# A fused convolution, low-rank mix and spectrum kernel: the second batch's convolution placed inside the first batch's blocks

## The reference

```python
# layer 1: causal convolution of 7 taps, the taps of each of 8 heads (24 channels) softmax-normalised
w = exp(weight - max); w = w / (sum(w) + 1e-9)
out[b, s, h] = sum_k w[h, k] * x_pad[b, s + k, h]
# layer 2: a low-rank mix over the positions (rank 32), then a two-layer network
u = x + (x^T @ U @ V)^T ;  x2 = u + relu(u @ w_ch1) @ w_ch2          # 192 -> 768 -> 192
# layer 3: real part of a 2-D Fourier transform over positions and channels, then again
mixed = real(fft(fft(x2, axis=1), axis=2)) ; u = x2 + mixed
un = (u - mean) / sqrt(var + 1e-6) ;  out = u + relu(un @ w_ch1') @ w_ch2'
```

## Time and profile before

| what | value |
| --- | --- |
| median of 3 runs | 1360.45 us (1359.39 to 1361.96) |
| the profiled execution | 1360.61 us, its span 1358.8 us |
| TensorE busy | 1301.7 us (96%) |
| VectorE busy | 940.5 us (69%) |
| ScalarE busy | 714.5 us (53%) |
| GpSimd busy | 470.7 us (35%) |

### The profile page before, as it was taken

The page is one execution under the profiler, slowest core; times in us unless marked ns, Lnnn a source line. Parts: engine busy times, 40 slices in busy tenths (PEclk is TensorE's granted clock), DMA queues, the critical chain, the costliest instruction groups (busy, mean ns, idle before and its releaser), DMA issues.

```text
span 1358.8 us, 25244 instructions
## 1 busy us (share of the span) xinstructions
PE 1301.7 (96%) x9128; PEld 1262.6 (93%) x9128; DVE 940.5 (69%) x2381; ACT 714.5 (53%) x1745; POOL 470.7 (35%) x611
## 2 busy tenths in 40 slices
PE   7799997859999999999999999999999999999998
PEld 7699996749999999999999999999999999999998
DVE  7857875755786886865788786875565666665554
ACT  5246653424565665654555665654444555555553
POOL 0001633550132474651133275561011234433332
PEclk9899997979999999999999999999999999999999
DMA  9842322113224323213224323311222222322220
GB/s 273 300 128 66 108 69 91 60 52 97 65 69 149 103 80 125 80 38 105 70 66 137 104 76 130 97 41 51 66 69 78 92 73 92 101 70 80 79 80 35
DMA packets 57757, 127.21 MB, mean 94 GB/s; under 512 B 8308, under 2 KB 24316, under 8 KB 55702
## 3 DMA queue, kind: packets, MB, share of 16 engines
q1 hardware_dynamic: 53602, 119.20, 27.9%
q0 software_dynamic: 4032, 6.41, 1.5%
HBM read 84.37 MB, written 46.77 MB: 97 GB/s over the span
## 4 chain that ended last, share of the span: by engine, by line
PE 80%; DVE 10%; ACT 3%; issue 3%; DMA 3%; POOL 2%; SPq 0%; POOLq 0%; ACTq 0%; DVEq 0%
PE bank L581 17%; PE bank L582 8%; PE bank L562 7%; PE bank L570 6%; PE bank L569 6%; PE bank L566 6%; PE bank L563 6%; PE bank L615 4%; PE bank L585 3%; DVE X L1069 3%; PE bank L638 3%; PE bank L630 2%; PE bank L629 2%; DMA vraw<-in_moe_V 2%; PE bank L628 1%
## 5 line engine op out<-in xcount | busy, mean ns | idle before, releaser
L776 ACT ACTIVATE ht<-bank 128x384 fp32r<-128x384 f32 x528 | 259.0, 490 | 467.1 <-PE bank L570 466.4
L982 DVE SCALAR_TENSOR_TENSOR ht<-bank,ht 128x384 fp32r<-128x384 f32 x528 | 293.3, 555 | 287.8 <-ACT ht L776 285.4
L581 PE MATMUL bank<-w,ht 128*128 128x384 f32 x1320 | 416.2, 364 | 5.5 <-DVE ub L990 3.5
L582 PE MATMUL bank<-w,ht 128*128 128x192 f32 x1320 | 331.0, 251 | 0.0
L1218 POOL TENSOR_TENSOR ub<-ub,tmp 128x576 f32<-128x576 f32 x88 | 125.7, 1429 | 589.9 <-DVE ub L990 438.9
L581 PEld LDWEIGHTS bank<-w,ht 128*128 128x128 f32 x1320 | 248.4, 188 | 12.7 <-issue 7.3
L582 PEld LDWEIGHTS bank<-w,ht 128*128 128x128 f32 x1320 | 252.0, 191 | 0.0
L562 PE MATMUL bank<-uth,w1h 128*128 128x384 f32 x528 | 189.2, 358 | 0.5 <-ACT uth L766 0.4
L570 PE MATMUL bank<-uts,w1t 128*128 128x384 f32 x528 | 180.4, 342 | 0.0
L569 PE MATMUL bank<-uts,w1s 128*128 128x384 f32 x528 | 179.9, 341 | 0.1
L566 PE MATMUL bank<-utl,w1h 128*128 128x384 f32 x528 | 179.5, 340 | 0.0
(11 more groups left out here) (115 smaller groups left out, 2562.5 us busy)
## 6 DMA issues: line engine op xcount, KB each, us to landing
f1t<-f_copy SPq DMA_DIRECT2D x44, 396.0 KB, 3.2
x_two<-ub SPq DMA_DIRECT2D x44, 288.0 KB
ub<-x_two SPq DMA_DIRECT2D x44, 288.0 KB, 3.1
mix<-mixed SPq DMA_DIRECT2D x44, 288.0 KB, 3.3
out<-ub SPq DMA_DIRECT2D x44, 288.0 KB
xin<-in_x SPq DMA_DIRECT2D x6, 1632.0 KB
vch<-v_split SPq DMA_DIRECT2D x44, 192.0 KB, 2.6
mixed<-rowk SPq DMA_DIRECT2D x88, 74.2 KB
```

Source lines behind the costliest of these rows:

```text
L581: e.matmul(dn[t][:, 0:2 * D], hh, w2[ph][:, m, :], start=(m == 0), stop=False)
L582: mm = e.matmul(dn[t][:, 0:D], hl, w2[ph][:, m, 0:D], start=False, stop=False)
L776: e.activation(hth[q % 4], up[q % 3][:, 0:TOK], ACT.Relu).then_inc(act_h, 1)
L982: e.scalar_tensor_tensor(htl[q % 4], up[q % 3][:, 0:TOK], 0.0, hth[q % 4].bitcast(F32), ALU.max, ALU.subtract).then_inc(dve_l, 1)
```

## The change

The second batch's convolution (c = 1) moves forward: piece 0 to steps (2,1) to (4,5), piece 1 to (6,1) to (8,5), piece 2 to (9,3) to (10,4) and groups 0 to 5 of the lone spectrum stage. Loads and T parts move with it. In the spectrum stage stand now also the split of T (group 10), the low-rank and make_u of block 11 (group 14) and its turn (group 16), which before came after the stage. The last block's output is added up by VectorE there instead of GpSimd. There are three row buffers instead of two. GpSimd's adds of a piece begin as soon as the first product that they need is in the plan (`late`), for all batches. At the start V's first split stands behind the third piece's taps on VectorE, V's second split is made by GpSimd after T's split, V's raw tile lies on the memory of `xin`, `prod` and `f1t` instead of the tiles of the blocks, SyncE stores the second half and loads `f1t` later, and VectorE makes five heads of the fourth piece instead of four.

```diff
-VEC_HEADS_0 = (5, 5, 4, 4)
+VEC_HEADS_0 = (5, 5, 4, 5)
...
-ROWS = 2
+ROWS = 3
...
+        T_LAST, LOW_AT, TURN_AT = 10, 14, 16
...
             if c == 1:
-                spots = [[(n, m) for n in range(n0 + 3, n0 + 7) for m in range(M6)],
-                         [(n, m) for n in range(n0 + 8, n0 + 11) for m in range(M6)],
-                         [("s", g) for g in range(3, NG)]]
-                loads = [(n0, 0), (n0 + 7, 0), ("s", 0)]
-                parts = [(n0 + 7, 3), ("s", 1), ("s", NG)]
+                span = lambda a, z: [(v // M6, v % M6) for v in range(a[0] * M6 + a[1], z[0] * M6 + z[1])]
+                spots = [span((2, 1), (5, 0)), span((6, 1), (9, 0)),
+                         span((9, 3), (10, 5)) + [("s", g) for g in range(6)]]
+                loads = [(0, 0), (5, 0), (9, 0)]
+                parts = [(5, 3), (9, 3), ("s", 8)]
...
# SyncE, start
+            store_v(0)
+            load_v(0)
+            load_v(1)
             e.wait_ge(pe_cv, len(PIECES_0))
-            e.wait_ge(ld_f1, 16)
-            load_f1(0)
-            load_f1(1)
             load_w2(1, w2b)
...
+            store_v(1)
+            e.wait_ge(ld_f1, 16)
+            load_f1(0)
+            load_f1(1)
...
# TensorE, spectrum_alone
-                for g in range(NG + 1):
+                for g in range(NG):
                     if ("s", g) in t_part:
                         part_of_t(*t_part[("s", g)])
+                    if g == LOW_AT:
+                        low_rank(NB)
+                    if g == TURN_AT:
+                        turn(NB)
                     if g + 2 < NG:
                         group_in(0, g + 2)
-                    if g < NG:
-                        group_out(0, g)
-                for q in range(4):
-                    e.wait_ge(tb_free[q], fills[("low", NB, 0)][1] if q == 0 else fills[("low", NB, 1)][1] if q == 1
-                              else filled[q])
+                    group_out(0, g)
+                for q in (2, 3):
+                    e.wait_ge(tb_free[q], filled[q])
...
# ScalarE: t_high(1) at group 10, turned_high(NB) at group 16
# VectorE, spectrum_alone
                 add_residual(NB - 1)
+                e.wait_ge(dve_y, NB * TB)
+                e.tensor_tensor(u_slot(NB - 1), u_slot(NB - 1), tmp[:], ALU.add).then_inc(pool_y, 1)
...
+                    if g == T_LAST:
+                        t_low(1)
+                    if g == LOW_AT:
+                        make_u(NB)
+                    if g == TURN_AT:
+                        turned_low(NB)
...
# VectorE, start
             start_taps(1)
-            v_low(0)
             start_taps(2)
-            v_low(1)
+            v_low()
             start_taps(3)
...
# GpSimd
-                late = -(-(VEC_HEADS + POOL_HEADS) * steps // (VEC_HEADS + PROD_OPS)) + 1
+                first = VEC_HEADS + POOL_HEADS
+                late = min(v for v in range(steps) if first in share(VEC_HEADS + PROD_OPS, v, steps, 0, 1))
...
+            e.wait_ge(v_h, 2)
+            e.wait_ge(dve_tst, 2)
+            vh = vout[2 * R:4 * R, :].rearrange("r (j p) -> r j p", p=128)
+            e.tensor_tensor(vh, vraw[2 * R:4 * R, :].rearrange("r (p j) -> r j p", j=N2)[:, 17:N2, :],
+                            vh.bitcast(F32), ALU.subtract).then_inc(v_l2, 1)
+            e.wait_ge(v_l2, 1)
```

More of the change, by code:

```diff
@@ L119, in program @@
         X = sb("X", [128, N2, D], F32)
+        with nc.sbuf_tensor("vraw", [4 * R, S], F32) as vraw:
+            pass
         xin = sb("xin", [128, PW + PAD, D], F32)
@@ L143, in program @@
         ident = sb("ident", [128, 128], F32)
-        with nc.sbuf_tensor("vraw", [4 * R, S], F32) as vraw:
-            pass
         uth = sb("uth", [128, 2, TOK], F32R)
@@ L290, in program @@
         for n in range(LAST + 1):
-            if n == 0 or previous(n) is None:
+            if n == 0:
                 fill_low(n)
@@ L309, in program @@
                     fill(("in", 0, g), (0, 2)[g % 2], True)
-                for g in range(NG + 1):
+                for g in range(NG):
                     if ("s", g) in t_part:
                         fill(("t",) + t_part[("s", g)], 0, False)
+                    if g == LOW_AT:
+                        fill_low(NB)
+                    if g == TURN_AT:
+                        fill_turn(NB)
                     if g + 2 < NG:
                         fill(("in", 0, g + 2), (0, 2)[g % 2], True)
-                    if g < NG:
-                        fill(("out", 0, g), (1, 3)[g % 2], True)
+                    fill(("out", 0, g), (1, 3)[g % 2], True)
         (ld_cw, ld_u, ld_id, ld_mir, ld_f1, ld_tab, ld_tabs, ld_v, ld_tail, ld_x, cw_ready, eps_set, halo_zero,
@@ L497, in store_rows, with store_v @@
                 e.dma_start(dst, rowk[:, (b * NG + g) % ROWS]).then_inc(row_out[(b * NG + g) % ROWS], 16)
-            for n, (a, z) in enumerate(((0, 17), (17, N2))):
+            def store_v(n):
+                a, z = ((0, 17), (17, N2))[n]
                 e.wait_ge((v_l, v_l2)[n], 1)
@@ L729, in _ @@
                 nx, pv = following(n), previous(n)
-                if pv is None:
+                if n == 0:
                     low_rank(n)
                     turn(n)
-                    if n == 0:
-                        e.wait_ge(w_l[0], 1)
+                    e.wait_ge(w_l[0], 1)
+                if pv is None:
                     up_slot(n, 0)
@@ L880, in spectrum_alone @@
                 for g in range(NG):
+                    if g == T_LAST:
+                        t_high(1)
+                    if g == TURN_AT:
+                        turned_high(NB)
                     if g + 2 < NG:
@@ L885, in spectrum_alone @@
                         conv_step(*conv[("s", g)])
-                t_high(1)
             e.wait_ge(cwc, 2)
@@ L934, in _ @@
             t_high(0)
-            e.wait_ge(v_l2, 1)
             e.wait_ge(v_stored, 16)
@@ L939, in _ @@
                 nx, pv = following(n), previous(n)
+                if n == 0:
+                    turned_high(n)
                 if pv is None:
-                    turned_high(n)
                     hidden(n, 0)
@@ L1093, in spectrum_alone @@
                 group_low(0, 1)
-                for g in range(NG + 1):
+                for g in range(NG):
                     if ("s", g) in t_part:
                         sum_t(*t_part[("s", g)])
+                    if g == T_LAST:
+                        t_low(1)
+                    if g == LOW_AT:
+                        make_u(NB)
+                    if g == TURN_AT:
+                        turned_low(NB)
                     if g + 2 < NG:
                         group_low(0, g + 2)
-                    if g < NG:
-                        group_rows(0, g)
+                    group_rows(0, g)
                     if ("s", g) in conv:
                         conv_step(*conv[("s", g)])
-                t_low(1)
             e.wait_ge(ld_cw, 16)
@@ L1133, in start_taps, with v_low @@
                         .then_inc(vec_cv, 1)
[L1135 to L1140 removed]
+            def v_low():
+                e.wait_ge(v_h, 1)
+                vh = ht[2 * R:4 * R, 0:17 * 128].rearrange("r (j p) -> r j p", p=128)
+                e.tensor_tensor(vh, vraw[2 * R:4 * R, :].rearrange("r (p j) -> r j p", j=N2)[:, 0:17, :],
+                                vh.bitcast(F32), ALU.subtract).then_inc(v_l, 1)
             def weights_low(n):
```

15 lines of the change are left out of this document (1 added, 14 removed).

## The result

The changed kernel takes 1364.1 us (median of 9 runs, 1362.2 to 1365.7) against 1359.2 for the kernel before (9 runs, 1357.0 to 1362.0): a ratio of 1.0032, 95% interval 1.0022 to 1.0043. Forecast were 1341.1 us in a range of 1332 to 1351. So it is slower, by a little more than can be told from none. The profiled execution took 1364.86 us, its span is 1363.0.

The account below looks back on a forecast made before the run. TensorE, busy 96% of the span, was taken as the bound, with gains only before 311 us. Terms -3.8 + 3.7 + 3.6 - 1.8 - 21.2 = -19.5 us from 1360.6 gave 1341.1 us, range 1332 to 1351.

Parts of the forecast that it names:

- Start: Before block 0: V's reordered splits let low-rank start at 59.4 instead of 63.26; -3.8 us (-7 to +1).
- T part: Blocks 0 to 10: one more part of T, 22 matmuls, lies where TensorE is the bound; +3.7 us.
- Convolution in the blocks: Blocks 0 to 10: denser convolution pieces make VectorE late for TensorE; +3.6 us (0 to +11).
- The rival of taking turns: VectorE and GpSimd operations wait for each other when both read SBUF tensors; total 1346 us, chance 0.17.
- Chain after the last block: Last down matmul to the DFT: less VectorE backlog, GpSimd's last add moved to VectorE; -1.8 us (-3.5 to +0.5).
- Spectrum stage: First spectrum matmul to block 12's low-rank: 59.1 us against 80.33; -21.2 us (-28 to -10).
- the six groups: Spectrum-stage groups with piece 2 of the convolution, put at 3.0 us each, 18 in all.
- the moved steps: Split of T, low-rank, make_u and turn inside the spectrum stage: 1.0 of TensorE, about 2 of waits; 3.0 us.
- The sixteen later groups: Spectrum-stage groups without convolution: a third row buffer brings them to 1.6 us each, 25.6 in all.
- Later batches: From 315 to 940 us: third row buffer and earlier adds lie under a busy TensorE; 0 (-1.5 to +1.5).
- The clock: Rival: gaps in TensorE lower its granted clock in blocks 2 to 10, adding 24 us; total 1365, chance 0.05.
- The point named for being wrong: Prediction counts as wrong if block spacing in 3 to 8 exceeds 14.5 us or late groups stay above 2 us.

Follow-up runs that it names:

- the kernel with all parts: Changed kernel with GpSimd's adds before its transfer, weight split in blocks 12 to 14, old add start for c > 1, block 11's low-rank/turn behind the groups: 1345.0 us.
- the spread kernel: The kernel with all parts, with piece 0 over 21 steps and piece 1 over 19 in place of 17, T parts in blocks 6 and 10: 1350.3 us.
- after: The changed kernel itself, all edits of the change against the kernel before: 1364.1 us, ratio 1.0032.
- the kernel with the steps inside: The kernel with all parts, but low-rank, make_u and turn of block 11 stay at groups 14 and 16 as in the changed kernel: 1353.6 us.
- the adds first: Changed kernel with GpSimd's convolution adds of a group placed ahead of that group's transfer of mirrored rows in the lone spectrum stage: 1354.3 us.

## Why the prediction was wrong, by its own steps

- *Start, -3.8.* Right in size and in what is late next: low-rank at 59.81, released by V's load (59.4 forecast). The store was issued 5.5 later and landed at 57.4, after 16.5 us. GpSimd's split took 5.53 (4.7 to 7.7) and cost nothing.
- *T part, +3.7.* Right: at 140.93 it takes 3.76 us. Block 5 with it takes 18.20 us, and 17.39 without GpSimd's long adds.
- *Convolution in the blocks, +3.6.* Failed, measured +9.7, inside its stated bounds of 0 to 11 (which add up to 11.9 as written). I put VectorE's operation at 0.64 us, the mean of the earlier trace rows, as if a denser piece left it there; it became 0.694, which is 3.7 us over 68 operations. The other 2.4 us are not measured one by one. The traces point to what an average hides: `lows` and the addition to `ub` stand in VectorE's queue behind single operations of 2 us and more, and TensorE waits for them (2.30 us at 181.13, 2.20 at 198.15, both released by VectorE's `ub`). The rival of taking turns, at 0.17, had the cause and only 0.8 us more for it.
- *Chain after the last block, -1.8.* Measured -0.7: VectorE's backlog of convolution, of which I had kept 1.0 us, is 1.3 (three operations at 226.89). The rest is not split up.
- *Spectrum stage, -21.2.* Failed, measured -9.5. Of the 11.7 us missing, 4.4 are the six groups (22.4 for 18.0): the sum counted GpSimd's work per group and not what stands behind what, and with the order on GpSimd changed they take 15.8. Another 2.2 are the last T part (5.94 for 3.7), which I priced at the full clock of the earlier trace rows, although the same part had taken 5.69 in the kernel before. The slow groups are not its whole reason: it takes 5.10 to 6.67 us in 17 of the 18 traces, 6.67 in the kernel with all parts, and 3.74 only in the spread kernel. 3.4 are the moved steps, put at 3.0 and 6.4 by their two gaps, and 1.6 the start of block 11, which is at half clock again. The sixteen later groups outside those gaps were right (1.14 to 2.01, mostly 1.46, for 1.6). That the third buffer makes them so was not: with two buffers they come nearly as fast, and the stage is 3.5 us longer.
- *Later batches, 0 (-1.5 to +1.5).* Failed, measured +4.65: 2.7 from the earlier adds and 1.7 at block 75, whose cause is open. A busy TensorE was taken to hide the adds; but it needs VectorE's `lows` in time, and these stand behind an operation that waits through three of GpSimd's.
- *The range.* The upper ends stated for the single terms add up to +7.7 us, 1368; the range ended at 1351. It took for granted that not several steps fail the same way at once.
- *The rivals.* Taking turns is right as a mechanism for the blocks and wrong in its price of 1346. Its 22.5 us for the six groups were met (22.4), but by luck: with GpSimd's adds cut to a column they still take 20.6, and with their order changed 15.8. The Trainium skill's lock ("SBUF — State Buffer", section "SBUF: two separate sides") agrees with the row of 1.99 us beside one subtraction of GpSimd's. The 3.56 us go beyond what it states: VectorE's operation began ahead of two of the three that it waited through. The clock fell in the spectrum stage; in the blocks it stayed at 1.00 in after's trace, but fell in block 8 or 9 in five other traces with the same blocks. The point named for being wrong was met, by block 8 with 16.01 us (blocks 3 to 7 take at most 14.53, block 5 less its T part 14.4). No case held six groups in one serial loop, and mending that loop won more than any other edit.

## What to carry to other kernels

When work of several engines is packed closer, write down for one round what stands behind what in each queue, and follow the ring of buffers once round: the sum of busy times per engine gave 3.0 us for a round that took up to 4.65. Where GpSimd reads SBUF beside it, allow that a VectorE operation with two SBUF inputs may last as long as a whole row of GpSimd's back-to-back operations (3.56 us for 0.49 here), and count for TensorE what stands behind it. Take the price of a piece of TensorE's work from a row at the clock that it will meet: two T parts of equal size took 3.73 and 5.69 us in one trace, before's. Test a compound edit part by part before judging it: here four details that lost 19 us stood in one change with the parts that won. And look at more than one trace before a difference of 2 to 4 us is given to an edit.

## What the runs showed of the hardware that was not expected

A VectorE operation of 0.49 us waited through three operations of GpSimd, 3.56 us in all, though GpSimd started two of them after it. ScalarE stood still with its input there, 3.36 and 2.35 us in the kernel with the steps inside, and in like gaps in four more of eighteen traces, all of two chips; kernels with the same ScalarE instructions had no such gap on another chip. TensorE's clock was at its lower level, 0.50, from 251.2 to 271.7 in after, beside a wait of 3.35 us, and at 0.96 on the mean of 243 to 260 with the adds first. It also fell in block 8 of that kernel (180.2 to 183.6), behind a wait of 2.28 us, where after's own trace, with a wait of 2.30, shows 1.00 throughout.
